# A fused retention, dense and mixture-of-experts kernel: dense blocks written out, nested end conditions, a weight piece in halves, flags read alone, two experts exchanged

## The reference

```python
state = gamma[None, :, None, None] * state + np.einsum('bhd,bhe->bhde', k[:, :, t], v[:, :, t])
y[:, :, t] = scale * np.einsum('bhd,bhde->bhe', q[:, :, t], state)
...
h = x @ w_in                                            # 3072 x 512 by 512 x 2048
g = np.maximum(h, 0.0) + np.log1p(np.exp(-np.abs(h)))
return (g @ w_out).astype(np.float32)
...
logits = x @ w_gate                                     # 8 experts
expert_idx = np.argmax(logits, axis=1)
...
    h = np.maximum(xe @ w1[e], 0.0)                     # 512 x 1024
    ye = h @ w2[e]                                      # 1024 x 512
    out[mask] = gate_w[mask, None] * ye
```

## Time and profile before

| | |
|---|---|
| median of 3 runs | 1026.38 us (1025.22 to 1027.52) |
| the profiled execution, its own time | 1027.39 us |
| its span in the profile | 1025.6 us |
| mean granted clock of TensorE | 0.992 |
| PE busy | 990.5 us (97%) |
| DVE busy | 508.9 us (50%) |
| ACT busy | 431.2 us (42%) |
| POOL busy | 159.7 us (16%) |

### The profile page before, as it was taken

One profiled execution on the slowest core, in us unless ns is written; L12 is line 12 of the kernel. 1 busy time (PEld: TensorE's weight loads), 2 busy tenths in 40 slices (PEclk: granted clock), 3 DMA queues, 4 the chain that ended last, 5 costly groups with the idle time before them and its releaser, 6 DMA issues.

```text
span 1025.6 us, 18900 instructions
## 1 busy us (share of the span) xinstructions
PE 990.5 (97%) x5968; PEld 855.7 (83%) x5969; DVE 508.9 (50%) x998; ACT 431.2 (42%) x755; POOL 159.7 (16%) x171
## 2 busy tenths in 40 slices
PE   6999999999999999999999999999999999999994
PEld 5888888888888888888888988887888888888773
DVE  3563465465366356366356587563223424345552
ACT  2655444444444444444444546333223323433541
POOL 3020010010011011011010002121222222233330
PEclk9999999999999999999999999999999999999998
DMA  9523211211111121021020014155111312453550
GB/s 349 181 84 123 72 43 42 69 46 42 50 65 42 32 82 42 24 82 51 13 86 16 32 42 144 52 204 207 42 41 45 118 51 73 165 197 121 186 214 12
DMA packets 28775, 91.89 MB, mean 90 GB/s; under 512 B 4062, under 2 KB 4190, under 8 KB 23584
## 3 DMA queue, kind: packets, MB, share of 16 engines
q1 hardware_dynamic: 23904, 76.48, 21.2%
q0 software_dynamic: 4800, 14.42, 4.3%
HBM read 78.30 MB, written 13.89 MB: 90 GB/s over the span
## 4 chain that ended last, share of the span: by engine, by line
PE 89%; DVE 3%; DMA 2%; ACT 2%; issue 2%; DVEq 1%; ACTq 0%; POOL 0%; SPq 0%; POOLq 0%
PE ps L1326 25%; PE ps L1311 25%; PE ps L1440 14%; PE ps L1415 14%; PE ps L1224 3%; PE ps L1232 2%; PE ps L1425 2%; PE ps L1249 1%; PE ps L1399 1%; PE ps L1241 1%; DMA arena<-w 1%; ACT W L684 1%; DMA arena<-w_out 1%; DVE W L1052 1%; DMA arena<-table 1%
## 5 line engine op out<-in xcount | busy, mean ns | idle before, releaser
L1311 PE MATMUL ps<-XS,W 128*128 128x384 f32 x1536 | 291.6, 338 | 6.6 <-DVE arena L828 2.6
L1326 PE MATMUL ps<-W,GS 128*128 128x512 f32 x1152 | 292.0, 397 | 2.3 <-DVE GS L832 2.2
L1311 PEld LDWEIGHTS ps<-XS,W 128*128 128x128 f32 x1536 | 273.0, 188 | 19.3 <-issue 3.4
L1326 PEld LDWEIGHTS ps<-W,GS 128*128 128x128 f32 x1152 | 211.3, 188 | 48.3 <-DVE GS L832 3.4
L1440 PE MATMUL ps<-W,XS 128*128 (+1 forms) x696 | 168.7, 399 | 5.8 <-DVE XS L1062 5.8
L1415 PE MATMUL ps<-W,XS 128*128 (+1 forms) x696 | 170.6, 394 | 0.0
L632 ACT ACTIVATE arena<-ps 128x384 f32<-128x384 f32 x128 | 62.9, 491 | 228.8 <-PE ps L1311 223.1
L1440 PEld LDWEIGHTS ps<-W,XS 128*128 128x128 f32 x696 | 130.7, 191 | 33.2 <-issue 6.7
L1415 PEld LDWEIGHTS ps<-W,XS 128*128 128x128 f32 x696 | 128.4, 188 | 25.6 <-DVE XS L1056 0.3
L828 DVE SCALAR_TENSOR_TENSOR arena<-ps,arena 128x384 f32<-128x384 f32 x128 | 71.1, 555 | 129.6 <-ACT arena L636 129.6
L843 DVE CUSTOM_DVE_ANT_0 arena<-arena 128x512 bf16<-128x512 f32 x168 | 129.1, 808 | 0.0
(11 more groups left out here) (163 smaller groups left out, 653.6 us busy)
## 6 DMA issues: line engine op xcount, KB each, us to landing
arena<-w SPq DMA_DIRECT2D x32, 1024.0 KB, 7.9
arena<-kT SPq DMA_DIRECT2D x24, 256.0 KB, 2.8
arena<-qT SPq DMA_DIRECT2D x24, 256.0 KB, 3.1
arena<-v SPq DMA_DIRECT2D x24, 256.0 KB, 4.1
arena<-k SPq DMA_DIRECT2D x24, 256.0 KB, 4.3
x_rows<-arena SPq DMA_DIRECT2D x24, 256.0 KB, 5.0
arena<-w_out SPq DMA_DIRECT2D x4, 1024.0 KB, 5.2
arena<-w_in SPq DMA_DIRECT2D x3, 1024.0 KB, 4.9
```

Of the source, the lines that this page charges most:

```text
L1311: last = pe.matmul(ps_h[g % 2], w_in_s[a][:, g // 4, k_, (g % 4) * P:(g % 4 + 1) * P], xs[half][b][:, k_, :], start=(k_ == 0 and a + b == ...
L1326: last = pe.matmul(ps_x[s], GS[:, g % 2, a, s * P:(s + 1) * P], w_out_s[b][:, g, :], start=(g == 0 and a + b == 0), stop=(g == GF - 1 and ...
```

## The change

Six edits are made together.

1. `ffn_blocks` writes all 8 dense blocks out; the loop is gone on all engines, and with it the waits against registers.
2. Piece 1 of the weights (the first of w_out) is split in two halves, the second of them at step 1 of the first block. Pieces 2 and 3 move from steps 1 and 3 to steps 2 and 4.
3. On PE the first `heads` of the first block moves from behind the third `strip_h` to behind the first one.
4. `steer` reads the flag alone; visit and parity are read within the condition, where there is a refill. Ahead of the loop DVE reads the flag of tile 4 before `scale_y`.
5. The conditions of the last tiles are nested: each lies within the one before.
6. The experts with turn 4 and 5 change places (three more steps in `first_expert`).

```diff
-PIECES_AT = [1, 3, 5, 7, 9, 11]
+PIECES_AT = [2, 4, 5, 7, 9, 11]
...
         def low_done(n):
-            return n + 2
+            return n + 3
...
-        def ffn_blocks(engine, one):
-            one(0, 0, True, True)
-            with engine.Fori(0, B - 1) as i:
-                one(i, 1, True, False)
-                one(i + 1, 0, True, False)
-            one(B - 1, 1, False, False)
+        def ffn_blocks(one):
+            for m in range(NBLK):
+                one(m // 2, m % 2, m < NBLK - 1, m == 0)
...
             x_high(0, 2, START_AT[2])
-            piece_high(1)
+            first_piece_high(2)
...
                     strip_high(n - 1, (g - 1) % 2)
+                    if first and g == 1:
+                        first_piece_high(3)
                     if first and g in PIECES_AT:
                         piece_high(2 + PIECES_AT.index(g))
...
             def steer(j):
-                return (act.value_load(refill_i[0:1, at1(j)], min_val=0, max_val=1),
-                        act.value_load(visit_i[0:1, at1(j)], min_val=0, max_val=E - 1),
-                        act.value_load(parity_i[0:1, at1(j)], min_val=0, max_val=1))
-            def refill(j, which, flag, visit, par):
+                return act.value_load(refill_i[0:1, at1(j)], min_val=0, max_val=1)
+            def refill(j, which, flag):
                 with act.If(flag > 0):
+                    visit = act.value_load(visit_i[0:1, at1(j)], min_val=0, max_val=E - 1)
+                    par = act.value_load(parity_i[0:1, at1(j)], min_val=0, max_val=1)
...
+                go(dve.tensor_scalar(of_first, turn_e, float(E // 2), None, ALU.is_equal))
+                done(dve.tensor_scalar(number, turn_e, float(E // 2 + 1), None, ALU.is_equal))
+                done(dve.tensor_tensor(turn_e, turn_e, of_first, ALU.add))
+                done(dve.tensor_tensor(turn_e, turn_e, number, ALU.subtract))
...
+            dve.wait_ge(s_tabs, 1)
+            flag = steer(TA)
             scale_y(TA - 1, 1, 16)
-            dve.wait_ge(s_tabs, 1)
-            refill(TA, 0, *steer(TA))
+            refill(TA, 0, flag)
...
             strip_h(0, 0, 0)
+            heads(0, SUB)
             strip_h(0, 0, 1)
-            ffn_blocks(pe, shifted)
+            ffn_blocks(shifted)
...
-            for j in range(NT0, NT):
+            def ending(j):
                 with pe.If(n_tiles > j):
                     tile(j - 1, (j - 1) % 2, 16 * ((j - 1) // 2 + 2), 2 if j + 1 < NT else 1)
+                    if j + 1 < NT:
+                        ending(j + 1)
+                        pe.sem_inc(s_left, 1)
+            ending(NT0)
```

More of the change, by code:

```diff
@@ L504, in one @@
                         decays(b, c0 + n)
-            ffn_blocks(pool, one)
+            ffn_blocks(one)
             bound = pool.to_reg(NTOK - 1)
@@ L747, in tile @@
                 if refills and ahead >= 1:
-                    refill(j - 1, 1, *before)
-                    refill(j + 1, 0, *after)
+                    refill(j - 1, 1, before)
+                    refill(j + 1, 0, after)
             for j in range(1, TA):
@@ L755, in _ @@
             act.wait_ge(s_tabs, 1)
-            refill(TA, 0, *steer(TA))
+            refill(TA, 0, steer(TA))
             with act.Fori(TA, NT0 - 1) as j:
@@ L760, in _, with ending @@
             final = act.value_load(ntile_i[0:1, 1:2], min_val=NT0 - 1, max_val=NT - 1)
-            for j in range(NT0, NT):
+            def ending(j):
                 with act.If(n_tiles > j):
                     tile(j - 1, 2 if j + 1 < NT else 1)
+                    if j + 1 < NT:
+                        ending(j + 1)
+                        act.sem_inc(s_left, 1)
+            ending(NT0)
             h_high(final)
@@ L1020, in shifted @@
                     strip_low(n - 1, (g - 1) % 2)
+                    if first and g == 1:
+                        first_piece_low(3)
                     if first and g in PIECES_AT:
@@ L1166, in steer, with refill @@
             def steer(j):
-                return (dve.value_load(refill_i[0:1, at1(j)], min_val=0, max_val=1),
-                        dve.value_load(visit_i[0:1, at1(j)], min_val=0, max_val=E - 1),
-                        dve.value_load(parity_i[0:1, at1(j)], min_val=0, max_val=1))
-            def refill(j, which, flag, visit, par):
+                return dve.value_load(refill_i[0:1, at1(j)], min_val=0, max_val=1)
+            def refill(j, which, flag):
                 with dve.If(flag > 0):
+                    visit = dve.value_load(visit_i[0:1, at1(j)], min_val=0, max_val=E - 1)
+                    par = dve.value_load(parity_i[0:1, at1(j)], min_val=0, max_val=1)
                     split_low(visit + 2, bass.ds(par, 1), which)
@@ L1199, in _, with ending @@
             final = dve.value_load(ntile_i[0:1, 1:2], min_val=NT0 - 1, max_val=NT - 1)
-            for j in range(NT0, NT):
+            def ending(j):
                 with dve.If(n_tiles > j):
                     tile(j - 1, (j - 1) % 2, 16 * ((j - 1) // 2), 2 if j + 1 < NT else 1)
+                    if j + 1 < NT:
+                        ending(j + 1)
+                        dve.sem_inc(s_left, 1)
+            ending(NT0)
             h_low(final)
@@ L1318, in strip_out @@
                 n = m * GF + g
-                if first and g % 4 == 0:
+                if first and g < 4 and g % 2 == 0:
+                    pe.wait_ge(s_wlo, 3 + g // 2)
+                elif first and g % 4 == 0:
                     pe.wait_ge(s_wlo, low_done(2 * (g // 4) + 1))
@@ L1456, in shifted @@
                     if attend:
-                        if a in A1_AT:
+                        if a in A1_AT and not (first and a == 0):
                             heads(b, c0 + A1_AT.index(a))
```

31 lines of the change are left out of this document (19 added, 12 removed).

## The result

The changed kernel takes 1020.34 us (median of 5 runs, 1019.65 to 1021.73), the kernel before 1025.55 on the same chip (5 runs, 1024.81 to 1027.52): ratio 0.9949, 95% interval 0.9934 to 0.9963. The profiled execution of the changed kernel took 1019.65 itself, its span is 1017.9 (before 1025.6): 7.7 us between the two profiles, 5.2 between the medians.

The account below looks back on a forecast made before the run. PE was taken as the bound wherever it has no idle time, so its late starts were priced: 3.1 - 1.5 + 3.9 + 1.3 - 2.6 + 2.9 = 7.1, 1020.3 against 1027.39, or 1019.3 from the median; range 1015 to 1023.5.

Parts of the forecast that it names:

- the better rival: Whole time 1015.5: loads ahead of the splits hidden (2.6), last `mm2` at full clock (1.4); 17 in 100.
- Start (3.1 gained): Start of the dense part: half piece shortens ACT's and DVE's chain, removing PE's gap and slow third strip; 3.1 us gained.
- Second `heads` (1.5 lost): First dense block: later piece 6 delays kT and qT of chunk 4, so PE's second `heads` waits 1.5 us.
- The sign "by 1 to 2 us": First dense block: the second `heads` should wait for a DMA by 1 to 2 us.
- Blocks (3.9 gained): Ends of the dense loop's passes: steps fall to 5.37 without branches back; 2.0 and 1.9, together 3.9 us gained.
- Tile 4 (1.3 gained): Ahead of tile 4: fewer register loads on DVE, so PE's gap of 1.32 goes altogether; 1.3 us gained.
- w1 splits (2.6 lost): Tiles 10, 16 and 19: two loads between `scale_y` and the split delay the next `mm2`; 2.6 us lost.
- The last tiles (2.9 gained): Expert part from tile 23 to the last: exchange, loads and nested conditions, summed by `mm2` starts; 2.9 us gained.
- 1.4 lost, then 1.2, 0.7 and 1.6 gained: Changes of the `mm2` steps to tiles 24, 25, 26 and 27, in that order, in us.
- Tile 24: `mm2(24)` over 13 behind the one before, since visit 6's w1 must be split in tile 23; 1.4 us lost.
- 0.65 at tile 26: `mm2(26)`: loads add 0.65 to the 13.45 behind a tile with two splits, giving 14.1 instead of 14.82.
- To the last tile (1.2 gained, part of the 3.7): Last `mm2`: one far jump hidden behind `mm2(27)`, DVE next late, 9.7 instead of 10.87; 1.2 us gained.

Follow-up runs that it names:

- early loads: Changed kernel with flag, visit and parity of a refill read together ahead of its condition, where the engine waits anyway; 1015.40 us against 1027.09, ratio 0.9883.
- The experiment with flat conditions: Changed kernel with PE's conditions of the last tiles one after another again instead of nested; 1021.04 us against 1027.09, ratio 0.9936.
- the kernel with the flags alone: Kernel before with refill flags read alone, visit and parity inside the condition, nothing else; 1027.76 us against 1025.98, ratio 1.0014.
- the second sitting: Changed kernel run again on another occasion, no edit; 1019.03 us against 1025.98 of the kernel before, ratio 0.9938.
- the kernel with the chunk first: Changed kernel with the early loads, and besides SP loads chunk 4 ahead of piece 6; 1014.83 us against 1025.66, ratio 0.9891.

## Why the prediction was right, and where it was not

The direction, the size and the range held. One sum of the prediction is off and nothing hangs on it: the better rival's terms, 2.6 and 1.4, give 1015.3 and not 1015.5. Of the three branches of L337 two were taken (3.71 and 3.33), and these agree with the rule on fetches; the third, of 0.08, was not. By steps:

- **Start (3.1 gained): measured 2.9 between the two first profiles,** but it is a sum of two things. The shorter chain is there always. The slow third strip, 1.2 of it, was a draw: it stands in three of five profiles with the old start (idle 2.12, 2.60 and 2.80), and not in the two with 2.17 and 1.37. Together with the second `heads` it gains 1.9 in the mean, from the first `strip_h` to the second block, where the prediction has 1.6.
- **Second `heads` (1.5 lost): right in mechanism, mis-sized.** The step takes 5.77 to 6.17 in five profiles instead of 5.37, 0.4 to 0.8 lost. POOL took up qT 6.7 after the issue of piece 6 (48.13 to 54.84), where the earlier trace rows gave 7.43: that is the 0.7 between forecast and trace. The issue of the piece and PE's own arrival (54.14) were each 1.0 later than forecast, which cancels. The sign "by 1 to 2 us" was not seen.
- **Blocks (3.9 gained): measured 3.87** in the two steps (7.38 and 7.23 to 5.37). Part b agrees in every pair of kernels without the early loads (3.2 to 4.5). The experiment that makes this edit alone shows it. By the branch of 108 ns of the Trainium skill (Advanced Engine Details and Errata, section Control Flow Timing) the edit would have brought 0.2; the runs disagree.
- **Tile 4 (1.3 gained): 1.56.**
- **w1 splits (2.6 lost): 2.5,** shown by two experiments, one that puts the loads there and one that takes them away.
- **The last tiles (2.9 gained): 3.7, but the exchange did not bring them.** This is the step that failed. For tiles 24 to 27 the forecast has 1.4 lost, then 1.2, 0.7 and 1.6 gained; the first profiles have 0.5 lost, then 1.2, 0.6 and 1.6 gained. Tile 24 is the term that was mis-sized: the weights were in time, and it came 12.71 behind, not over 13. The prediction credits the exchange with the sum of these, 2.1, and charges edit 4 with 0.65 at tile 26. The runs show that edit 4 alone shortens the four tiles from 54.4 and 54.1 to 51.4, and that the exchange beside it adds nothing. The place is tile 25 of the kernel before. The second piece of its split waits for a late transfer, and behind that piece six loads stood on DVE's path, 1.67 of them unhidden in the second profile; with edit 4 two are left and hidden, PE's gap falls from 2.1 or 2.3 to 0.2 and the clock stays. The prediction took the six loads behind a split as hidden but for 0.28, which the earlier trace rows show for a split whose weights are in time, and did not ask what they cost behind a late one.
- **Luck in the same step.** The forecast is reckoned against a profile with the late transfer. Where it came sooner, in the kernel with the blocks written out, the four tiles took 50.5, which is 0.9 less than in the changed kernel. How often it is late was not measured; it was in both profiles of the kernel before.
- **To the last tile (1.2 gained, part of the 3.7): 1.05** (10.86 to 9.81, 9.7 forecast), the next late is DVE as forecast. The experiment with flat conditions has 10.39, 0.6 above. The other 0.5 is the length of the branches: its two far ones take 5.63 together, those of the first profile of before 6.11. In the five profiles with flat conditions they take 5.6 to 6.7 and the step 10.4 to 11.5, most of all in the kernel with the flags alone, so fewer loads on DVE are not what shortens it. The nesting gives 0.6 to 1.7, by how long the branches are in an execution.

Why 7.7 between the profiles and 5.2 between the medians: the profiled execution of before (1027.39) was near its slowest run (1027.52), and that of the changed kernel was its fastest. Profiles of the same program differ by 1.2 in part a, by 1.6 to tile 27 and by 1.4 in part d. In the kernel before the 1.2 is the slow third strip; in the changed kernel it is 0.5 of an earlier first strip and 0.3 at the second `heads`, the rest spread. The 1.6 is a slow stretch behind an idle time of about two us, and the 1.4 goes with a longer one behind the last gap (its `mm2(28)` took 7.10 and 8.50). In the second sitting the medians were 7.0 apart, the ratio gives 6.4, the second profiles 6.6. The forecast's 7.1 lies above the middle of both sittings and inside the second's interval.

## What to carry to other kernels

Where loads of registers steer an engine that is on the path, what counts is where they stand: ahead of work that another engine waits for they cost their length, behind a wait that is there anyway nothing. Reading fewer of them at a worse place lost 3.1 us at four tiles and gained 4.2 to 4.9 at others, the larger part only where a transfer was late; reading all of them at the right place took 5.2 to 7.0 us more from the expert part, about as much as the whole change had brought.
An order of work that moves a stall from one tile to the next should be costed over all the tiles that it touches; here, beside edit 4, it was worth nothing.
When single steps are worth one us and the time of one execution varies by as much, cut the span in parts and profile the same program twice before a difference is explained.

## What the runs showed of the hardware that I had not expected

**The clock can fall with no idle time at all.** In the three kernels with the loads early a slow stretch begins at 645.0 to 645.5, and in none of the nine other profiles, with no idle time of PE in the profile ahead of it. The stretches around it, of the kernel with the chunk first (PE, PEld, DVE, ACT, POOL busy with counts, granted clock, DMA share, GB/s):

```profile
640.00:645.40 5.40, 5.40 (x44) 5.07 (x44) 1.37 (x5) 1.14 (x3) 1.21 (x2) 1.00 0.11 22
645.40:648.90 3.50, 3.50 (x11) 2.72 (x10) 3.16 (x14) 1.16 (x3) 0.00 (x0) 0.51 0.10 41
```

PE was busy for all of the 5.40 us ahead, 2.74 of them with 24 matmuls of 8 columns, the router's:

```profile
641.87 2.74 PE L1389 MATMUL ps<-gate_k,arena 128*128 128x8 f32 x24
...
645.30 4.58 PE L1449 MATMUL ps<-W,XS 128*128 128x512 f32 x12
```

The `mm1` behind them took 4.58 where the next one took 3.00: 1.6 us. The same matmuls stand there in all kernels; why the clock falls in these three is open.

**The length of an idle time doesn't decide by itself whether the clock falls.** It fell after idle 1.81, 2.07, 2.12, 2.32, 2.60 and 2.80, and stayed after 1.37, 1.74 and 2.17. (The last tile is left out: two gaps follow each other there, and the clock fell in all twelve profiles.) So a gap near two us costs itself or itself and 1.2 to 1.6 more, in the same code. A group that reads 7.3 us is not at the lower clock throughout: of the 7.33 of `mm2(26)` in the kernel before, 3.4 were at granted clock 0.50, the rest at 1.00.

**A far branch taken lasts 2.7 to 4.1 us on PE's sequencer** (23 of them in the twelve profiles); a near or untaken one 0.07 to 0.36. The same branch of the same program took 2.90 and 3.24 in the two profiles of the kernel before. The branch of 3.51 us cost the changed kernel nothing while PE still had a `mm2` in its queue. The Trainium skill, Runtime: NRT & Kernel Launch, section Instruction fetch mechanics, says that a taken branch out of the window of loaded code waits for a fetch; the long branches here agree, their length is from the rows.
